# Two q buffers taken in turn, and x0 read back two places later

## The chip, the cores and the metric

One core of a Trainium2 chip runs the whole program. A core has five engines that run their own instruction streams and meet only at semaphores: TensorE (PE in the rows) multiplies matrices, VectorE (DVE), ScalarE (ACT) and GpSimd (POOL) work elementwise, and SyncE (SP) only issues the transfers (DMA) between DRAM and the on-chip memory here. The metric is the device time of one execution in microseconds (us), median of the runs.

## The reference

An attention over pooled keys feeds two feed-forward layers:

```
k_p, v_p = means of k and v over groups of 8 rows       # 8 x 8 heads, 576 rows, 64 wide
attn = softmax(q @ k_p^T / 8);  x = attn @ v_p          # x: 4608 tokens x 512
h = x @ w_in;    g = max(0.01 h, h);         x1  = g @ w_out     # 512 -> 2048 -> 512
h = x1 @ w2_in;  g = h * clip(h+3, 0, 6)/6;  out = g @ w2_out
```

All of it is float32. Each float32 matrix product is made of three products of rounded parts (high by high, high by low, low by high).

## The kernel before, in words

**Tiles, steps and places.** The tokens are cut into 9 tiles of 512 columns for each of the two layers, 18 tiles in all. A tile is worked off in 8 steps, each for two blocks of the hidden layer. The first matrix product of a step (`part`, L1393) is done by seven smaller block products, numbered 0 to 6; the eight matmul groups of the second product (`second`, L1421) that belong to earlier steps lie between them. Each step has 8 places, so a tile has 64. The attention of the next batch runs between these matmuls, at fixed places: tile 0 to tile 6 each carry the four units (pairs of heads) of one batch. A unit's nine stages stand in the table `UNIT_PLACES`: its scores (q times the pooled k) stand second, at the places 3, 15, 27 and 39 for the units 0 to 3; `pv1`, the last, gives the last half of its x0.

**SP's queue.** SP issues all transfers in program order, and waits in order too: a transfer that waits holds all behind it. In an attention tile (`attention_tile`, L509) this order is written out place by place. `stream` (L455) reloads the ring buffer of a weight factor once the product that used it is done, for use two steps later. At LOAD_PLACES `load_unit` (L392) loads k, q and v of the next unit; q's load waits until the scores of the unit before have been multiplied, because all units after the first batch share one q buffer. At STORE_PLACES `store_x0` (L396) stores a unit's x0 to DRAM, and at X_PLACES `load_x0` (L406) reads the columns of the tile to come back into x_stage, after waiting for the store to land. After step 1 `store_y` stores the four banks of the tile before.

**The second layer's weights.** In the tiles 2 to 6 the kernel also prepares the second layer's weight factors, seven in each tile: ScalarE rounds a factor (`factor2_hi`, L873, at places 19 to 25), GpSimd takes the rest (L766), and SP stores it (`store_prep2`, L478, at places 21 to 27). The buffer stage2 has four slots, so that factor 4 uses slot 0 again, once the store of factor 0 has landed:

```
act.wait_ge(prep2_stored[at % SLOTS2], stored2(i, at))
nc.scalar.activation(stage2[:, at % SLOTS2, 0:2], ...)
```

Behind it on ScalarE, in step 3, stands the copy of product 0 out of the accumulator (`p`, L1045), for which product 2 waits on TensorE, since it uses the same bank.

Of the kernel before, what the change touches and what calls it, by code (L numbers as in the profile page):

```python
# [11 lines left out]
P = 128  # L12
# [5 lines left out]
ROWS = 96  # L18
SUB = S // ROWS
HALF_SUB = SUB // 2  # L20
HALF = S // 2
# [28 lines left out]
LOAD_PLACES = (3, 15, 27, 39)  # L50
STORE_PLACES = (16, 28, 40, 51)
X_PLACES = (18, 30, 42, 53)

FIRST_UNIT_PLACES = [(0, 6, 7, 9, 10, 13, 15, 16, 18),
# [3 lines left out]
FIRST_LOAD_PLACES = (6, 19, 30, 41)  # L58
FIRST_STORE_PLACES = (20, 31, 42, 52)
FIRST_X_PLACES = (22, 33, 44, 54)  # L60


SUM_K_PLACES = (52, 10, 22, 34)
# [72 lines left out]
def ffn_attention_kernel(nc, qT, kT, v, w1_in, w1_out, w2_in, w2_out, x0T, x1T, w1_in_split,  # L136
                         w2_in_split, out):
    with ExitStack() as ctx:
        def sb(name, shape, dt=F32):
            return ctx.enter_context(nc.sbuf_tensor(name, shape, dt))  # L140
# [4 lines left out]
        def sem(name):  # L145
            return ctx.enter_context(nc.semaphore(name))
# [7 lines left out]
        def attention_buffers(sb, c, pad=0):  # L154
            def buf(name, shape, dt=F32):
                return sb(name + str(c), shape, dt)
            u = AttentionBuffers()
            if pad:
                buf("pad", [P, pad // 4])
            u.k_raw = buf("k_raw", [P, KEYS, POOL])  # L160
            u.v_raw = buf("v_raw", [KEYS, 2, D, POOL])
            u.q_raw = buf("q_raw", [P, 2, HALF])
            u.k_sum = buf("k_sum", [P, KEYS])
            u.v_sum = buf("v_sum", [KEYS, 2, D])
            u.kT = buf("kT", [P, PAIR_KEYS])
            if c:
                buf("gap", [P, 4 * HALF + PAIR_KEYS])
            u.v_hi = buf("v_hi", [KEYS, 2, P], F32R)
            u.v_lo = buf("v_lo", [KEYS, 2, P], F32R)
            u.prob = buf("prob", [ROWS, 2, HALF_SUB * 2, KEYS])  # L170
            u.row_max = buf("row_max", [ROWS, 2, HALF_SUB * 2])
            u.row_sum = buf("row_sum", [ROWS, 2, HALF_SUB * 2])
            u.row_den = buf("row_den", [ROWS, 2, HALF_SUB * 2])
            u.row_inv = buf("row_inv", [ROWS, 2, HALF_SUB * 2])
            u.pT_hi = buf("pT_hi", [KEYS, 2, HALF], F32R)
            u.pT_lo = buf("pT_lo", [KEYS, 2, HALF], F32R)
            u.x0_stage = buf("x0_stage", [P, 2, HALF])
            return u
# [4 lines left out]
        units = [None] * PAIRS  # L183
# [3 lines left out]
        for c, groups in ((1, (0, 2)), (2, (1, 3))):  # L187
            ring.append(sb(f"ring{c}", [P, PRODUCTS, 4, P], F32R))
            units[c] = overlaid(lambda sb: attention_buffers(sb, c, 4096))
            for group in groups:  # L190
                w_hi = sb(f"wout_hi{group}", [P, ROWS_IN, DM], F32R)
                wout_raw[group] = overlaid(lambda sb: sb(f"wout_raw{group}", [P, ROWS_IN, DM]))
                wout[group] = [w_hi, sb(f"wout_lo{group}", [P, ROWS_IN, DM], F32R)]
        units[3] = overlaid(lambda sb: attention_buffers(sb, 3, 128))
        p1, u2, u3 = (sb(name, [P, HN]) for name in ("p1", "u2", "u3"))
        h = sb("h", [P, 2, N])
# [9 lines left out]
        raw = overlaid(lambda sb: sb("raw", [P, 2, 4, 2, P]))  # L206
        y_stage = sb("y_stage", [P, DC, N])
        units[0] = attention_buffers(sb, 0, 32)
        xp_hi = overlaid(lambda sb: (sb("pad_hi", [P, 3, 2, HN]),
                                     sb("xp_hi", [P, DC, N], F32R)))[1]  # L210
# [15 lines left out]
        def first(b):  # L226
            return isinstance(b, int) and b == 0

        def buffers(b, c):
            return units[c] if first(b) else units[0]  # L230

        def freed(b, c):

            return 0 if first(b) else PAIRS * b + c

        def per_pair(name):
            return [sem(name + str(c)) for c in range(PAIRS)]
# [9 lines left out]
        q_loaded = per_pair("q_loaded")  # L247
# [7 lines left out]
        scores_done = sem("scores_done")  # L255
# [106 lines left out]
        def above_zero(eng, semaphore, value):  # L362

            if not isinstance(value, int) or value > 0:
                eng.wait_ge(semaphore, value)
# [7 lines left out]
        def is_first(T):  # L373
            return isinstance(T, int) and T == 0
# [4 lines left out]
        def _(sp):  # L379
            def load_k_q(b, c):  # L380

                u = buffers(b, c)
                above_zero(sp, k_summed, freed(b, c))
                sp.dma_start(u.k_raw[:], kT[b, c]).then_inc(k_loaded[c], 16)
                above_zero(sp, scores_done, 2 * freed(b, c))
                sp.dma_start(u.q_raw[:], qT[b, c]).then_inc(q_loaded[c], 16)

            def load_v(b, c):
                above_zero(sp, v_summed, freed(b, c))
                sp.dma_start(buffers(b, c).v_raw[:], v[b, c]).then_inc(v_loaded[c], 16)  # L390

            def load_unit(b, c):  # L392
                load_k_q(b, c)
                load_v(b, c)

            def store_x0(b, c):  # L396
                sp.wait_ge(x0_copied, 2 * (PAIRS * b + c) + 2)
                sp.dma_start(x0T[c * P:(c + 1) * P, bass.ds(b * S, S)],
                             buffers(b, c).x0_stage[:].rearrange("p a n -> p (a n)")
                             ).then_inc(x0_stored[c], 16)  # L400
# [87 lines left out]
            def attention_at(T, place, next_unit=True):  # L488
                loads, stores, x_loads = (
                    (FIRST_LOAD_PLACES, FIRST_STORE_PLACES, FIRST_X_PLACES) if is_first(T)  # L490
                    else (LOAD_PLACES, STORE_PLACES, X_PLACES))
                for c in range(PAIRS):
# [41 lines left out]
            sp.wait_ge(first_k_summed, 1)  # L534
            sp.dma_start(units[0].k_raw[:], kT[1, 0]).then_inc(k_loaded[0], 16)
            sp.wait_ge(scores_done, 2)
            sp.dma_start(units[0].q_raw[:], qT[1, 0]).then_inc(q_loaded[0], 16)
            store_x0(0, 0)
            store_x0(0, 1)
            load_piece(0)  # L540
# [306 lines left out]
        def _(act):  # L847
# [39 lines left out]
            def piece_hi(piece):  # L887
                _, raw_w, hi, _ = piece_views(piece)
                act.wait_ge(w_loaded[piece % PIECES], 16 * (piece // PIECES + 1))
                nc.scalar.activation(hi, raw_w, ACT.Copy).then_inc(w_hi_ready, 1)  # L890
# [475 lines left out]
        def _(pe):  # L1366
            def product(acc, left, right, first=True, last=True):

                pe.matmul(acc, left[0], right[0], start=first, stop=False)  # L1369
                pe.matmul(acc, left[0], right[1], start=False, stop=False)  # L1370
                return pe.matmul(acc, left[1], right[0], start=False, stop=last)  # L1371
# [73 lines left out]
            def stage(name, b, c):  # L1445
                u, n = buffers(b, c), 4 * b + c
                if name == "scores":
                    pe.wait_ge(q_loaded[c], 16 * (b + 1))
                    pe.wait_ge(kT_ready, 2 * n + 2)
                    above_zero(pe, x0_copied, 2 * freed(b, c))  # L1450
                    for half in range(2):
                        for at in range(HALF_SUB):
                            mm = pe.matmul(
                                u.ps[0:ROWS, half, at * PAIR_KEYS:(at + 1) * PAIR_KEYS],
                                u.q_raw[:, half, at * ROWS:(at + 1) * ROWS], u.kT[:],
                                start=True, stop=True)
                        mm.then_inc(scores_done, 1)
                if name in ("turn_p0", "turn_p1"):
                    half = int(name[-1])
                    pe.wait_ge(prob_ready, 2 * n + half + 1)  # L1460
                    for hd in ((0, 1), (1, 0))[half]:
                        if half == 1 and hd == 0:
                            pe.wait_ge(x0_copied, 2 * n + 1)
                        for j in range(HALF_SUB):
                            mm = pe.transpose(u.ps[0:KEYS, hd, j * ROWS:(j + 1) * ROWS],
                                              u.prob[:, half, 2 * j + hd, :],
                                              ident[0:ROWS, 0:ROWS])
                    mm.then_inc(p_turned, 1)
                if name in ("pv0", "pv1"):
                    half = int(name[-1])  # L1470
                    pe.wait_ge(pT_ready, 2 * n + half + 1)
                    if half == 0:
                        pe.wait_ge(v_ready, 2 * n + 2)
                    for hd in range(2):
                        mm = product(u.ps[:, half, 0:HALF], (u.v_hi[:, hd, :], u.v_lo[:, hd, :]),
                                     (u.pT_hi[:, hd, :], u.pT_lo[:, hd, :]), hd == 0, hd == 1)
                    mm.then_inc(pv_done, 1)
# [134 lines left out]
```

## Time and profile before

| what | value |
|---|---|
| time, median of 3 runs | 1733.42 us (1729.87 to 1739.12) |
| the profiled execution: time, span | 1732.34 us, 1730.6 us |
| mean granted clock of TensorE | 0.992 |
| TensorE busy | 1691.3 us (98% of the span) |
| VectorE, ScalarE, GpSimd busy | 1024.0, 632.5, 394.1 us |
| DMA | 366.04 MB on SP's queue, 67.3% of 16 engines |

The span runs from the first to the last instruction of the profiled execution. Busy TensorE is not TensorE at its peak, as its matmuls overlap. Attention fills roughly the first 790 us, then tiles run without it.

### The profile page before, as it was taken

To read this page: it belongs to the slowest core of one execution; us is meant where nothing else is said; L and a number is where in the kernel's file an instruction comes from. 1 tells how busy PE (TensorE), PEld (TensorE's weight loads), DVE (VectorE), ACT (ScalarE), POOL (GpSimd) and SP (SyncE) were. 2 spreads that over 40 slices of the span, in tenths; PEclk is the share of its full clock that TensorE was granted. 3 is DMA by queue.
4 is the path that set the end of the run, shared out by engine and by line. 5 is a ranking of instruction groups with operands and counts; after the bars stand their busy time and mean duration, and the time that the engine had idled before them with its cause. 6 is when DMAs were issued, how large, how long until landed. Compare 5 with 4: busy or idle time off the path is not lost. (4 is left out here: it accounts for less than half of the span.)

```text
span 1730.6 us, 33189 instructions
## 1 busy us (share of the span) xinstructions
PE 1691.3 (98%) x10588; PEld 1506.7 (87%) x10588; DVE 1024.0 (59%) x1807; ACT 632.5 (37%) x1329; POOL 394.1 (23%) x427
## 2 busy tenths in 40 slices
PE   7999999999999999999999999999999999999999
PEld 6788888988888888899999888989898888989898
DVE  7767776686766867666454655454544444444444
ACT  4554443333333433333222333333333333333332
POOL 6226542021120212103332202121211112121200
PEclk8999999999999999999999999999999999999999
DMA  7756877667676676767777757575757675757562
GB/s 199 228 159 201 271 249 247 214 201 259 204 243 220 208 247 215 242 196 268 239 258 245 257 172 224 176 220 175 218 170 220 178 219 171 223 173 223 173 197 77
DMA packets 215810, 366.83 MB, mean 212 GB/s; under 512 B 22464, under 2 KB 47040, under 8 KB 215744
## 3 DMA queue, kind: packets, MB, share of 16 engines
q1 hardware_dynamic: 215744, 366.04, 67.3%
q8 instruction: 30, 0.49, 0.1%
q14 instruction: 36, 0.29, 0.0%
HBM read 308.28 MB, written 57.67 MB: 211 GB/s over the span
## 5 line engine op out<-in xcount | busy, mean ns | idle before, releaser
L1416 PE MATMUL ps_h<-xs_hi,ring 128*128 128x256 f32 x3808 | 823.8, 285 | 20.5 <-ACT p L1045 15.9
L1416 PEld LDWEIGHTS ps_h<-xs_hi,ring 128*128 128x128 f32 x3808 | 645.5, 190 | 69.5 <-ACT p L1045 19.8
L1416 PE MATMUL ps_h<-xs_lo,ring 128*128 128x256 f32 x1904 | 537.4, 282 | 0.0
L1416 PEld LDWEIGHTS ps_h<-xs_lo,ring 128*128 128x128 f32 x1904 | 361.2, 190 | 27.0
L931 ACT ACTIVATE g_hi<-gate 128x512 fp32r<-128x512 f32 x288 | 181.9, 632 | 404.6 <-DVE gate L1126 221.8
L1185 DVE TENSOR_TENSOR u<-ps_h,p 128x256 f32<-128x256 f32 x272 | 114.2, 420 | 205.9 <-PE ps_h L1416 155.0
L1369 PE MATMUL ps_y<-g_hi,wout_hi 128*128 128x512 f32 x576 | 229.2, 398 | 0.5 <-DVE y_stage L1181 0.3
L1370 PE MATMUL ps_y<-g_lo,wout_hi 128*128 128x512 f32 x576 | 228.7, 397 | 0.0
L1370 PE MATMUL ps_y<-wout_lo,g_hi 128*128 128x512 f32 x576 | 227.8, 395 | 0.0
L1369 PE MATMUL ps_y<-wout_hi,g_hi 128*128 128x512 f32 x576 | 227.5, 395 | 0.1
L1371 PE MATMUL ps_y<-g_hi,wout_lo 128*128 128x512 f32 x576 | 226.1, 393 | 0.0
L1371 PE MATMUL ps_y<-wout_hi,g_lo 128*128 128x512 f32 x576 | 224.3, 389 | 0.0
L923 ACT ACTIVATE pre<-h,three 128x512 f32<-128x512 f32 x144 | 103.2, 717 | 265.1 <-DVE h L1185 206.6
L1185 DVE TENSOR_TENSOR h<-ps_h,u 128x256 f32<-128x256 f32 x272 | 113.8, 418 | 101.3 <-PE ps_h L1416 100.8
L747 POOL TENSOR_TENSOR xs_lo<-x_stage,xs_hi 128x512 fp32r<-128x512 f32 x30 | 43.9, 1464 | 492.6 <-ACT xs_hi L903 492.6
L1145 DVE SCALAR_TENSOR_TENSOR g_lo<-gate,g_hi 128x512 fp32r<-128x512 f32 x144 | 103.9, 722 | 85.4 <-ACT g_hi L931 85.4
L1132 DVE SCALAR_TENSOR_TENSOR gate<-pre,h 128x512 f32<-128x512 f32 x144 | 109.5, 760 | 66.1 <-ACT pre L923 66.0
L1141 DVE TENSOR_TENSOR g_lo<-gate,g_hi 128x512 fp32r<-128x512 f32 x144 | 106.8, 742 | 62.3 <-ACT g_hi L931 60.7
L1371 PEld LDWEIGHTS ps_y<-g_hi,wout_lo 128*128 128x128 f32 x576 | 108.9, 189 | 24.3
L1371 PEld LDWEIGHTS ps_y<-wout_hi,g_lo 128*128 128x128 f32 x576 | 108.3, 188 | 23.9
L1369 PEld LDWEIGHTS ps_y<-g_hi,wout_hi 128*128 128x128 f32 x576 | 109.4, 190 | 8.8 <-DVE y_stage L1181 0.8
L1126 DVE SCALAR_TENSOR_TENSOR gate<-h 128x512 f32<-128x512 f32 x144 | 108.5, 754 | 13.0 <-ACT h L1007 4.2
(115 smaller groups left out, 2021.4 us busy)
## 6 DMA issues: line engine op xcount, KB each, us to landing
ring<-w_in_split SPq DMA_DIRECT2D x920, 256.0 KB, 2.8
w_in_split<-ring SPq DMA_DIRECT2D x56, 256.0 KB, 3.6
w_in_split<-stage SPq DMA_DIRECT2D x56, 256.0 KB, 4.3
k_raw<-in_kT SPq DMA_DIRECT2D x32, 288.0 KB, 3.4
q_raw<-in_qT SPq DMA_DIRECT2D x32, 288.0 KB, 3.1
v_raw<-in_v SPq DMA_DIRECT2D x32, 288.0 KB
x0T<-x_stage SPq DMA_DIRECT2D x32, 288.0 KB, 4.4
x1T<-y_stage SPq DMA_DIRECT2D x36, 256.0 KB, 3.8
```

The source lines that it names most:

```text
L747: nc.gpsimd.tensor_tensor(xs_lo[:, r], x_block(r), xs_hi[:, r].bitcast(F32), ALU.subtract).then_inc(x_ready, 1)
L923: nc.scalar.activation(pre[:, upper], h[:, upper], ACT.Relu, bias=three[:]).then_inc(pre_ready, 1)
L931: nc.scalar.activation(g_hi[:, g_slot(i, upper)], gate[:, upper], ACT.Copy, scale=1.0 / 6.0 if layer == 2 else 1.0).then_inc(g_hi_ready, 1)
L1126: nc.vector.scalar_tensor_tensor(gate[:, upper], h[:, upper], SLOPE, h[:, upper], ALU.mult, ALU.max).then_inc(gate_ready, 1)
L1132: nc.vector.scalar_tensor_tensor(gate[:, upper], pre[:, upper], 6.0, h[:, upper], ALU.min, ALU.mult).then_inc(gate_ready, 1)
L1141: nc.vector.tensor_tensor(g_lo[:, slot], gate[:, upper], g_hi[:, slot].bitcast(F32), ALU.subtract).then_inc(g_ready, 1)
L1145: nc.vector.scalar_tensor_tensor(g_lo[:, slot], gate[:, upper], 1.0 / 6.0, g_hi[:, slot].bitcast(F32), ALU.mult, ALU.subtract).then_inc(g_ ...
L1185: return nc.vector.tensor_tensor(to, banks[bank], other, ALU.add)
L1369: pe.matmul(acc, left[0], right[0], start=first, stop=False)
L1370: pe.matmul(acc, left[0], right[1], start=False, stop=False)
L1371: return pe.matmul(acc, left[1], right[0], start=False, stop=last)
L1416: mm = pe.matmul(banks[BANK_OF[r]], a, b[:, r, c, :], start=r in OPENS and c == 0 and n == 0, stop=c == 1 and n == 2, skip_group_check=True)
```

## The change

The batch-by-batch units get two q buffers, taken in turn by unit number; with them the load of q waits for the scores of the unit two before instead of those of the unit before. The reload of x0 is placed two places later for the units 0 to 2 of a tile (the last stays at 53). In tile 0 the loads of units move one or two places up, and the reloads of x0 two places down.

```diff
-X_PLACES = (18, 30, 42, 53)
+X_PLACES = (20, 32, 44, 53)
...
-FIRST_LOAD_PLACES = (6, 19, 30, 41)
+FIRST_LOAD_PLACES = (4, 18, 29, 40)
...
-FIRST_X_PLACES = (22, 33, 44, 54)
+FIRST_X_PLACES = (24, 35, 46, 54)
...
-            u.q_raw = buf("q_raw", [P, 2, HALF])
+            u.q_raw = [buf(f"q_raw{i}_", [P, 2, HALF]) for i in range(1 if c else 2)]
...
+        def q_of(b, c):
+            return buffers(b, c).q_raw[0 if first(b) else c % 2]
...
-                above_zero(sp, scores_done, 2 * freed(b, c))
-                sp.dma_start(u.q_raw[:], qT[b, c]).then_inc(q_loaded[c], 16)
+                if not first(b):
+                    sp.wait_ge(scores_done, 2 * (freed(b, c) - 1))
+                sp.dma_start(q_of(b, c)[:], qT[b, c]).then_inc(q_loaded[c], 16)
...
-                                u.q_raw[:, half, at * ROWS:(at + 1) * ROWS], u.kT[:],
+                                q_of(b, c)[:, half, at * ROWS:(at + 1) * ROWS], u.kT[:],
```

SP's queue in tile 6 before, from the q load at place 15 to the first three factor stores (places 21 to 23). x1T is where y is stored, x0T where x0 goes and comes from, w2_in_split takes the factors of the second layer:

```order
L386 DMA q_raw0<-in_qT 128x576 [waits scores_done]
L390 DMA v_raw0<-in_v 72x1024 [waits v_summed]
L470 DMA x1T<-y_stage 128x512 [waits y_copied_act]
L470 DMA x1T<-y_stage 128x512 [waits y_copied_dve]
L470 DMA x1T<-y_stage 128x512 [waits y_copied_act]
L470 DMA x1T<-y_stage 128x512 [waits y_copied_dve]
L452 DMA ring1<-w1_in_split 128x512 [waits product_done] x2
L398 DMA x0T<-x0_stage0 128x576 [waits x0_copied]
L452 DMA ring1<-w1_in_split 128x512 [waits product_done] x2
L403 DMA x_stage<-x0T 128x512 [waits x0_stored0,x_ready]
L452 DMA ring1<-w1_in_split 128x512 [waits product_done] x3
L480 DMA w2_in_split<-stage2 128x512 [waits prep2_ready] x3
```

The same piece of the queue in the changed kernel:

```order
L392 DMA q_raw0_0<-in_qT 128x576 [waits scores_done]
L396 DMA v_raw0<-in_v 72x1024 [waits v_summed]
L476 DMA x1T<-y_stage 128x512 [waits y_copied_act]
L476 DMA x1T<-y_stage 128x512 [waits y_copied_dve]
L476 DMA x1T<-y_stage 128x512 [waits y_copied_act]
L476 DMA x1T<-y_stage 128x512 [waits y_copied_dve]
L458 DMA ring1<-w1_in_split 128x512 [waits product_done] x2
L404 DMA x0T<-x0_stage0 128x576 [waits x0_copied]
L458 DMA ring1<-w1_in_split 128x512 [waits product_done] x4
L409 DMA x_stage<-x0T 128x512 [waits x0_stored0,x_ready]
L458 DMA ring1<-w1_in_split 128x512 [waits product_done]
L486 DMA w2_in_split<-stage2 128x512 [waits prep2_ready] x3
```

Four ring loads instead of two now stand between the store of x0 and its reload, and one instead of three between the reload and the factor stores. The q load has the same place and another value to wait for.

SP's queue at the start of tile 0 before:

```order
L431 DMA w1_in_split<-ring2 128x512 [waits block_ready] x3
L384 DMA k_raw0<-in_kT 128x576 [waits k_summed]
L386 DMA q_raw0<-in_qT 128x576 [waits scores_done]
L390 DMA v_raw0<-in_v 72x1024 [waits v_summed]
L420 DMA raw<-in_moe_w_in 128x2x128 [waits block_ready]
```

And in the changed kernel:

```order
L388 DMA k_raw0<-in_kT 128x576 [waits k_summed]
L392 DMA q_raw1_0<-in_qT 128x576 [waits scores_done]
L396 DMA v_raw0<-in_v 72x1024 [waits v_summed]
L437 DMA w1_in_split<-ring2 128x512 [waits block_ready] x3
L426 DMA raw<-in_moe_w_in 128x2x128 [waits block_ready]
```

The three stores of weight blocks now stand behind the loads of k, q and v.

## Rows read from the trace of the kernel before

**Rows 1.** Busy time by stretch (PE, PEld, DVE, ACT, POOL), granted clock, DMA share, GB/s.

```profile
180.00:283.00 103.00, 101.50 (x664) 89.96 (x663) 79.10 (x137) 41.07 (x100) 47.63 (x56) 1.00 0.77 251
...
283.00:800.00 517.00, 503.26 (x3266) 450.16 (x3265) 361.18 (x660) 181.21 (x426) 84.30 (x109) 0.99 0.71 225
800.00:1731.00 931.00, 922.46 (x5740) 826.70 (x5738) 452.46 (x812) 323.60 (x611) 177.74 (x143) 1.00 0.65 203
```

**Rows 2.** Timeline of PE, the five waits: start, us, instruction, [idle before <-releaser].

```profile
298.94 0.39 PE L1416 MATMUL ps_h<-xs_hi,ring 128*128 128x256 f32 x1 [3.10 <-ACT p L1045]
...
405.15 0.40 PE L1416 MATMUL ps_h<-xs_hi,ring 128*128 128x256 f32 x1 [2.44 <-ACT p L1045]
...
511.54 0.58 PE L1416 MATMUL ps_h<-xs_hi,ring 128*128 128x256 f32 x1 [2.38 <-ACT p L1045]
...
618.36 0.38 PE L1416 MATMUL ps_h<-xs_hi,ring 128*128 128x256 f32 x1 [3.07 <-ACT p L1045]
...
722.78 0.56 PE L1416 MATMUL ps_h<-xs_hi,ring 128*128 128x256 f32 x1 [2.14 <-ACT p L1045]
```

**Rows 3.** Stretches behind the first, fourth and fifth wait: PE busy, clock, DMA.

```profile
299.00:303.00 4.00, 4.00 (x17) 0.57 0.79 284
...
618.00:622.00 4.00, 3.49 (x21) 1.00 0.78 245
722.00:727.00 5.00, 4.21 (x17) 0.66 0.74 239
```

**Rows 4.** Timeline of ACT: the rounding of factors 4 and 5.

```profile
298.20 0.42 ACT L883 ACTIVATE stage<-s_sum 128x256 fp32r<-128x256 f32 x1 [4.03 <-DMA w_in_split<-stage]
...
301.18 0.40 ACT L883 ACTIVATE stage<-s_sum 128x256 fp32r<-128x256 f32 x1
```

**Rows 5.** Timeline of SP's transfers from place 15 to place 23 of tile 2.

```profile
277.20 1.28 SPq L384 DMA_DIRECT2D k_raw<-in_kT  x1
281.11 0.34 SPq L386 DMA_DIRECT2D q_raw<-in_qT  x1
...
282.18 2.27 SPq L470 DMA_DIRECT2D x1T<-y_stage  x4
...
286.53 0.34 SPq L398 DMA_DIRECT2D x0T<-x_stage  x1
287.01 1.11 SPq L452 DMA_DIRECT2D ring<-w_in_split  x2
291.39 0.35 SPq L403 DMA_DIRECT2D x_stage<-x0T  x1
291.86 1.31 SPq L452 DMA_DIRECT2D ring<-w_in_split  x3
293.42 1.54 SPq L480 DMA_DIRECT2D w_in_split<-stage  x3
```

**Rows 6.** Timeline of PE: last matmul of products 5 and 6, transposes before the wait.

```profile
288.10 0.28 PE L1416 MATMUL ps_h<-xs_hi,ring 128*128 128x256 f32 x1
...
290.04 0.28 PE L1416 MATMUL ps_h<-xs_hi,ring 128*128 128x256 f32 x1
...
295.18 0.66 PE L1465 MATMUL ps_att<-ident,prob 96*72 96x96 f32 x6
```

**Rows 7.** Timeline of POOL: the low parts of factor 0, and of factors 1 and 2.

```profile
286.27 0.74 POOL L766 TENSOR_TENSOR stage<-raw_s,stage 128x256 fp32r<-128x256 f32 x1
290.65 1.93 POOL L766 TENSOR_TENSOR stage<-raw_s,stage 128x256 fp32r<-128x256 f32 x2 [3.64 <-ACT stage L883]
```

**Rows 8.** Timeline of DVE: the sum of v at place 13.

```profile
277.59 1.21 DVE L1248 TENSOR_REDUCE v_sum<-v_raw 72x128 f32<-72x1024 f32 x1
```

**Rows 9.** Busy time by stretch, as rows 1.

```profile
280.00:282.00 2.00, 2.00 (x19) 2.00 (x18) 1.49 (x3) 0.18 (x1) 0.00 (x0) 1.00 0.12 44
```

**Rows 10.** Line L480, the factor stores issued at 293.42 and at 300.69: landing times.

```profile
DMA to landing us min/median/max: 4.8/4.8/4.8
...
DMA to landing us min/median/max: 2.9/2.9/2.9
```

More of the change, by code:

```diff
@@ L536, in _ @@
             sp.wait_ge(scores_done, 2)
-            sp.dma_start(units[0].q_raw[:], qT[1, 0]).then_inc(q_loaded[0], 16)
+            sp.dma_start(q_of(1, 0)[:], qT[1, 0]).then_inc(q_loaded[0], 16)
             store_x0(0, 0)
```

## The prediction, made before the changed kernel ran

> **What bounds the kernel now.** I read the stages first, by busy time in stretches [rows 1]. After the attention part (800 to 1731 us) TensorE is busy for 922.5 of 931 us at full clock. The change touches no instruction there, so I take that stretch as fixed. In the attention part TensorE is again what counts: in 180 to 283, one tile's length, it is idle for 1.5 us of 103; in 283 to 800, five tiles' length, for 13.7 us of 517, at a mean clock of 0.99. ScalarE and VectorE are far from full there. So only a wait that TensorE itself feels, or a lowered clock, is worth time.
>
> Then I read what TensorE waits for between 283 and 800 us. There is one long wait in each of the five tiles 2 to 6, always at the same point: the first matmul of product 2 in step 3 of the tile waits for ScalarE's copy p (L1045): 3.10, 2.44, 2.38, 3.07 and 2.14 us [rows 2]. These are 13.1 of the 13.7 us. Behind the first wait, the clock is granted at 0.57 for 4 us, that is three of four microseconds near the lower level (1.2 instead of 2.4 GHz), a loss of 4 x 0.43 = 1.7 us. Behind the second and third the rows read the same (three such in all); behind the fifth 5 us show 0.66 (5 x 0.34 = 1.7 us); behind the fourth, though it was one of the longest, the clock stayed at 1.00 [rows 3]. Four losses of 1.7 are 6.8 us. The place is worth 13.1 + 6.8 = 19.9 us.
>
> Why is p late? ScalarE runs in order, and ahead of p it rounds factor 4 of the second layer's weights into a slot of stage2 (L883). Four slots serve seven factors, so factor 4 needs slot 0, whose old content must have been stored to DRAM. ScalarE is idle for 4.03 us until that store has landed, at 298.20; then it rounds, copies p, then TensorE at 298.94 [rows 4]. Had the store landed 3.10 us earlier, at 295.10, TensorE would not have waited: its transposes before it end at 295.84 [rows 6].
>
> Why does the store land late? Its data were ready at 287.01 (GpSimd, 286.27 + 0.74) [rows 7], but SP issued it only at 293.42 [rows 5], over six microseconds later. SP's queue says why. At place 15 it issues k at 277.20, and the next instruction, q, only at 281.11: it waits for the scores of the unit before, at the same place in TensorE's order. It then pushes v and four y stores, so ring loads and the store of x0 follow late and bunched: x0's store goes out at 286.53. Two ring loads later, SP meets the reload of x0, which waits for that store; it stands until 291.39. Only then come three ring loads in a row, whose products had all ended by 290.32 (290.04 + 0.28) [rows 6], and then the store that ScalarE needs.
>
> **The change part by part.**
> *Two q buffers.* The load of q now waits for the scores of the unit two before, which lie twelve places back, some 19 us at 103 us for 64 places. At place 15 SP gets q out right behind k, near 278.6 instead of 281.11. The v load needs the sum of the v before it, which is placed at 13; that sum ends at 278.80 (277.59 + 1.21) [rows 8], so v goes near 279. Then y (2.27 us; its last bank is copied in step 1 as well, at place 10) to about 281.7, the first two ring loads of step 2, and the x0 store near 283.5 instead of 286.5, its data being copied behind place 14. The transfers don't crowd: in 280 to 282 the DMA engines are busy only 0.12 of the time now [rows 9]. No instruction is added on any engine; SP has the same count of transfers. In the Fori loop two register operations move, and none of TensorE's do.
> *The x0 reload two places later* (18 to 20). SP issues the ring loads of products 3, 4 and 5 as they end, and meets the reload after product 5, whose matmuls end at 288.38 [rows 6]. The x0 store, out at 283.5, has then had 4.9 us; in before it took no more than 4.9 us (286.53 to 291.39 [rows 5]). So the wait is about nothing. The reload goes at 288.8; its data aren't needed before all four pieces are there, and the fourth stays at place 53, so this costs nothing. The ring load of product 6 then waits for its product, 290.32, takes 0.1 + 0.36 us, and the factor store follows 0.25 us behind (as from 291.86 + 1.31 to 293.42 in [rows 5]): 291.0 instead of 293.42, that is 2.4 us earlier. It can't be earlier, since product 6 stands ahead of it.
> *When it lands.* In before the landing took 4.8 us, behind one x0 load and three ring loads issued in 2 us; a later store of the same size with little ahead of it took 2.9 us [rows 10]. The two ends are landings at 293.9 and at 295.8. By the first nothing is left of the wait. By the second 295.8 - 295.1 = 0.7 us is left in each of the two tiles with a 3.1 us wait and none in the other three: 1.4 us. I take a point between, 0.5 us in all, since two instead of four transfers stand just ahead.
> The Trainium skill (DMA: Bandwidth & Descriptors, section Queues, rings and completion order) speaks against this part: the increment of a semaphore is a strongly ordered write, which lands only after every earlier write of the same DMA engine. The trace agrees in kind: 4.8 us with a queue ahead and 2.9 us with little. By this rule the reload, now right ahead of the factor store, is itself part of its landing, which pulls toward the longer of my two ends.
> *The same move in units 2 and 3 (30 to 32, 42 to 44) and the earlier q* free SP of waits too, but ring loads are issued two steps (over 20 us) before their use and TensorE waits for none of them, so I count 0. If that cover were gone, every microsecond of a late ring load would show on TensorE.
> *Tile 0.* Loads of k, q, v come one or two places earlier, one set now ahead of three weight stores instead of behind; the x0 reloads go two places later. TensorE has no SP-fed wait there. 0, bounded by +-2 us, the size of the idle time before 283.
> *Behind the wait.* With the pause gone, factors 5 and 6 need slots 1 and 2. Factor 1 is ready in GpSimd before 292.6 [rows 7], its store goes out near 292, and even at 4.8 us it lands before 297; ScalarE reaches factor 5 at 301.18 now [rows 4], less 3.1 us that is 298.1. So no stall follows there.
>
> **Sum.** The waits 13.1 - 0.5 = 12.6, the clock 6.8: 19.4 us. The profiled execution took 1732.34 us (span 1730.6), 1 us under the median of the runs, 1733.42; I predict 1732.3 - 19.4, rounded to 1713 us. By the bounds: 18.5 us to 19.9 us, and +-2 us for tile 0 and the luck of the clock.
>
> **The rivals.**
> *Half of it.* The store lands 5 to 6 us after its issue because reload, ring load and the traffic moved forward are still under way. With 0.8 us more than the 4.8, the waits left are 1.5, 0.8, 0.8, 1.5 and 0.5 us, 5.1 us in all, and if the clock still falls behind them as before, only 8.0 us are won: 1724 us. For it: DMA share near full in this stretch now. Against it: that share is high because SP pushes a backlog, which the change spreads.
> *Nothing.* SP is held by something else behind q (the v sum, the y copies, or ring products), or the store is not what p waits for: 1732 us. Against it: SP's queue runs nearly without pause from 281.11 to 288.1, so it was working off a backlog.
> *Slower.* The pause is where ScalarE and VectorE catch up. Without it, the softmax chain of the following units (probabilities, turned and split) comes late for TensorE at the places 25 to 60. Each such wait would cost what one of today costs, about 2.6 + 1.4 = 4 us. One new wait per tile gives the gain back (5 x 4 = 20 us, no change); from two per tile on it is slower, by 20 us: 1753 us. For it: VectorE is busy 361 of 517 us, in bursts. Against it: the stretch 180 to 283 has the same softmax work and no such pause, VectorE is busy for 79.1 of its 103 us, and TensorE is idle for 1.5 us [rows 1].
>
> **How the numbers follow.** Forecast (1713, own range 1709 to 1719): 0.76. Half: 0.11, split between faster and same. Nothing, or gain given back: 0.08. Slower: 0.05. Within 0.5% (8.7 us) a measurement of this kernel can't tell a change. Faster 0.76 + 0.08 = 0.84, same 0.11, slower 0.05. The range reaches from 1708 (all of the 19.9 us, 2 us of tile 0, and a better draw of the clock) to 1727.
>
> **What would show it.** On SP: q right behind k at places 3, 15, 27, 39; no wait over 1 us at the x0 reload of unit 0; the first factor store 2 to 2.5 us after where TensorE's product 5 ends, not 5. On ScalarE: the wait of factor 4 for the store under 1 us. On TensorE: no wait for p over 1 us in tiles 2 to 6, and their mean clock 1.00. Tiles 2 to 6 should take about 4 us less each, all else the same. I am wrong if the factor store is issued early and ScalarE still waits for its landing, or if TensorE's waits come back on the turned probabilities.

## The result, and the profile after

The changed kernel takes 1713.67 us, median of 4 runs (1712.43 to 1718.73), against 1734.09 us for the kernel before: a ratio of 0.9887, 95% interval 0.9853 to 0.992. The forecast was 1713. Timed again later beside other kernels it took 1714.41 us, ratio 0.9878 (0.9858 to 0.9899).

The stretches of the changed kernel (columns as in [rows 1]):

```profile
250.00:800.00 550.00, 548.54 (x3601) 490.58 (x3600) 401.56 (x726) 199.40 (x466) 103.10 (x128) 1.00 0.74 234
800.00:1717.00 917.00, 908.68 (x5655) 814.28 (x5653) 443.70 (x800) 320.08 (x602) 169.90 (x135) 1.00 0.65 202
```

The same first stretch of the kernel before:

```profile
250.00:800.00 550.00, 535.87 (x3478) 479.08 (x3477) 388.52 (x708) 193.36 (x452) 89.89 (x115) 0.99 0.70 224
```

TensorE's idle time there fell from 14.1 to 1.5 us and the clock is full. The five waits of [rows 2] are gone. All that the list of waits gives for TensorE between 250 and 800 us, in the kernel after:

```profile
PE ps_h L1422 <- DVE h L1191: 0.9, 3, 0.3
```

(0.9 us in three waits, the longest 0.3.) SP's queue at place 15 to 21 of tile 2, as in [rows 5]:

```profile
282.99 0.75 SPq L388 DMA_DIRECT2D k_raw<-in_kT  x1
283.93 0.34 SPq L392 DMA_DIRECT2D q_raw<-in_qT  x1
284.62 0.33 SPq L396 DMA_DIRECT2D v_raw<-in_v  x1
285.23 2.52 SPq L476 DMA_DIRECT2D x1T<-y_stage  x4
287.91 1.24 SPq L458 DMA_DIRECT2D ring<-w_in_split  x2
289.41 0.34 SPq L404 DMA_DIRECT2D x0T<-x_stage  x1
289.90 4.63 SPq L458 DMA_DIRECT2D ring<-w_in_split  x4
294.87 0.35 SPq L409 DMA_DIRECT2D x_stage<-x0T  x1
296.15 0.32 SPq L458 DMA_DIRECT2D ring<-w_in_split  x1
296.73 0.34 SPq L486 DMA_DIRECT2D w_in_split<-stage  x1
```

And ScalarE at the same place, as in [rows 4]:

```profile
299.43 0.54 ACT L959 ACTIVATE kT<-k_sum 64x72 f32<-64x72 f32 x2
300.23 0.42 ACT L889 ACTIVATE stage<-s_sum 128x256 fp32r<-128x256 f32 x1 [0.26 <-DMA w_in_split<-stage]
300.55 0.36 ACT L1051 ACTIVATE p<-ps_h 128x256 f32<-128x256 f32 x1
```

In this execution the tile lies 5.79 us later than in the profile before (k at 282.99 instead of 277.20). With that taken off, q goes out at 278.1, the x0 store at 283.6, the reload at 289.1 without a wait of note, and the factor store at 290.9 instead of 293.42. It lands 3.5 us later (300.23 - 296.73), and ScalarE waits for it 0.26 us instead of 4.03.

The 5.79 us come from the prologue, and they hide a part of the gain in the profiled pair (1718.73 against 1732.34 us, 13.6 us apart). Counted from the load of k at place 15 of tile 2 to the end of the span, the pair is 1730.6 - 277.20 = 1453.4 and 1716.9 - 282.99 = 1433.9 us: 19.5 us apart. The first 75 us, before, then after, then in the run with the late reload alone (further down), whose program is that of before up to tile 1:

```profile
0.00:75.00 75.00, 61.64 (x360) 53.24 (x361) 53.27 (x86) 36.50 (x81) 36.68 (x68) 0.91 0.72 214
```

```profile
0.00:75.00 75.00, 62.18 (x334) 54.48 (x335) 52.36 (x84) 34.71 (x75) 31.87 (x64) 0.82 0.68 218
```

```profile
0.00:75.00 75.00, 62.24 (x334) 54.58 (x335) 52.52 (x84) 34.72 (x75) 31.94 (x64) 0.82 0.70 214
```

TensorE is busy about as long, at a lower clock: 75 x 0.09 = 6.8 us less of full-speed time. SP's order in the changed kernel differs from about 48 us on (tile 0), but the third line shows the same low clock with the order of before, and tile 2 lies 4.99 us late there too. So it is in the main a matter of the single execution; the section on surprises has more of them.

### The profile page after: what moved, and what is told of

The parts are those of the page before. It is cut to its first block and busy times, and to the rows that moved or that the text cites. A ratio compares the mean times of both kernels' runs of the same rounds, so it can differ in the third digit from the quotient of the medians.

```text
span 1716.9 us, 33189 instructions
## 1 busy us (share of the span) xinstructions
PE 1690.1 (98%) x10588; PEld 1505.8 (88%) x10588; DVE 1026.2 (60%) x1807; ACT 632.3 (37%) x1329; POOL 395.4 (23%) x427
## 5 line engine op out<-in xcount | busy, mean ns | idle before, releaser
L1132 DVE SCALAR_TENSOR_TENSOR gate<-h 128x512 f32<-128x512 f32 x144 | 108.7, 755 | 13.7 <-ACT h L1013 4.9
```

The costliest lines, as they stand in the source:

```text
L1132: nc.vector.scalar_tensor_tensor(gate[:, upper], h[:, upper], SLOPE, h[:, upper], ALU.mult, ALU.max).then_inc(gate_ready, 1)
```

## The experiments

My theory: product 6 and SP's position in its queue decide when the store of factor 0 goes out; that store decides when ScalarE rounds factor 4; and the copy p behind it decides whether TensorE waits. Rivals: the reload alone counts; the traffic, not the issue, makes the landing late; the gain comes from elsewhere. The executions of a kernel spread over 2 to 13 us, so medians are compared by their ratios to the runs of before that they share.

**The two q buffers alone.** The edit is against the changed kernel; it sets all three tables of places back to those of before.

```diff
-X_PLACES = (20, 32, 44, 53)
+X_PLACES = (18, 30, 42, 53)
...
-FIRST_LOAD_PLACES = (4, 18, 29, 40)
+FIRST_LOAD_PLACES = (6, 19, 30, 41)
...
-FIRST_X_PLACES = (24, 35, 46, 54)
+FIRST_X_PLACES = (22, 33, 44, 54)
```

> The two q buffers alone, every place as in the kernel before. Queue theory: SP gets q, v and y out 2.5 us earlier at place 15, the store of x0 goes out near 3 us earlier and has landed some 3 us earlier, so the reload at place 18 frees SP by about 288.4 (before: 291.39), the ring loads of products 4 and 5 go at once, product 6 sets the factor store, which is issued about 2.4 us earlier: all of the gain of the full change, about 19 us (1714). Rival, that moving the reload is what counts: less than 6 us (over 1727), with TensorE's five waits for p still over 1.5 us each.

Measured 1716.36 us, ratio 0.988 (0.9863 to 0.9898): the gain of the full change within what can be told. SP:

```profile
288.24 0.34 SPq L404 DMA_DIRECT2D x0T<-x_stage  x1
288.72 1.10 SPq L458 DMA_DIRECT2D ring<-w_in_split  x2
292.55 0.35 SPq L409 DMA_DIRECT2D x_stage<-x0T  x1
293.01 1.78 SPq L458 DMA_DIRECT2D ring<-w_in_split  x3
295.05 2.18 SPq L486 DMA_DIRECT2D w_in_split<-stage  x3
```

SP still stands at the reload, from 289.8 to 292.55, but that ends early enough: product 6 is what it waits for last, and the store goes out 2.5 us earlier than before, by the tile's own time (this tile lies 4.12 us later). It lands 4.4 us behind its issue, ScalarE waits 1.19 us for it, and TensorE's waits for p are 0.5 us in all the tiles together.

**The late reload alone.** The edit is against the kernel before.

```diff
-X_PLACES = (18, 30, 42, 53)
+X_PLACES = (20, 32, 44, 53)
```

> One q buffer; the reloads of x0 two places later in the tiles 1 to 6 (20, 32, 44), tile 0 as before. Queue theory: SP is still behind until 288.1, sends two more ring loads, then stands at the reload until the x0 store lands at 291.4, and issues the first factor store near 292.3, 1.1 us earlier. The five waits shrink by 1.1 us each, 5.5 us in all, to 2.0, 1.3, 1.3, 2.0, 1.0; if the clock still falls behind them about 1727, if it no longer does, 1721. Rival, that moving the reload carries the gain: 1714.

Measured 1727.93 us, ratio 0.9945 (0.9927 to 0.9963). The five waits for p are smaller, not gone:

```profile
302.38 0.39 PE L1416 MATMUL ps_h<-xs_hi,ring 128*128 128x256 f32 x1 [1.55 <-ACT p L1045]
...
407.11 0.39 PE L1416 MATMUL ps_h<-xs_hi,ring 128*128 128x256 f32 x1 [2.01 <-ACT p L1045]
...
512.37 0.39 PE L1416 MATMUL ps_h<-xs_hi,ring 128*128 128x256 f32 x1 [1.69 <-ACT p L1045]
...
617.55 0.39 PE L1416 MATMUL ps_h<-xs_hi,ring 128*128 128x256 f32 x1 [1.53 <-ACT p L1045]
...
721.04 0.38 PE L1416 MATMUL ps_h<-xs_hi,ring 128*128 128x256 f32 x1 [1.09 <-ACT p L1045]
```

They are 7.9 us in all where 7.6 were expected. The store goes out at 296.76, which is 291.8 by the times of before (this tile lies 4.99 us later): 1.6 us earlier where 1.1 was expected, and it lands 4.9 us behind its issue. The clock fell behind the second and the third wait only (stretches behind the second, the third and the fifth; PE busy, clock, DMA):

```profile
408.00:412.00 4.00, 4.00 (x18) 0.61 0.49 160
513.00:517.00 4.00, 4.00 (x17) 0.57 0.75 214
...
723.00:727.00 4.00, 3.91 (x26) 1.00 0.84 248
```

Two losses near 1.7 us remain of four. They stand behind the two longest waits of this run (2.01 and 1.69 us), but both waits are shorter than the one of 3.07 us in the kernel before behind which the clock stayed full [rows 3]. Each part of the change works on the same wait, so their gains, by the ratios 0.0120 x 1735 = 20.8 us and 0.0055 x 1735 = 9.5 us, don't add up: both together give 20 us.

**The reload behind the factor stores, one q buffer.** The edit is against the kernel before.

```diff
-X_PLACES = (18, 30, 42, 53)
+X_PLACES = (24, 30, 42, 53)
```

> One q buffer; only the first reload of x0 of a tile is moved, from place 18 to 24, behind the first four factor stores; q still waits for the scores of the unit before. Queue theory: nothing stands between SP and the factor store but the products, so it goes out near 291.0 although q, v and y leave as late as before: 1714, waits for p under 0.7 us. Rival, that the burst of q, v, y and ring transfers (DMA share near 1.0 from 284 to 290) makes the store land late whenever it is issued: the landing takes over 6 us and less than half of the gain is seen (over 1724).

Measured 1715.04 us, ratio 0.9877 (0.986 to 0.9894). One number of one table does what the whole change does. q still waits for its scores and y leaves late, and yet:

```profile
283.96 0.34 SPq L386 DMA_DIRECT2D q_raw<-in_qT  x1
...
289.95 3.58 SPq L452 DMA_DIRECT2D ring<-w_in_split  x5
293.79 2.18 SPq L480 DMA_DIRECT2D w_in_split<-stage  x3
```

The store goes out 2.5 us earlier than before (this tile lies 2.86 us later). It lands 4.7 us behind its issue (ScalarE rounds factor 4 at 298.52), so the traffic does lengthen the landing, as it did before (4.8 us, [rows 10]); it doesn't cost the gain. The rival needed over 6 us. TensorE's waits for p are 0.7 us in all. Medians can't tell this kernel or the one with q alone from the changed one. The single profiles hint at a rest: from the load of k at place 15 of tile 2 to the end of the span they take 1435.7 and 1436.5 us, the changed kernel 1433.9 and, timed again, 1432.9.

**The stores taken off SP's queue.** ScalarE issues all seven of a tile at the same places; q and x0 are untouched. The edit is against the kernel before.

```diff
-                if 0 <= place - STORE2_PLACE < PRODUCTS:
-                    store_prep2(i, place - STORE2_PLACE)
...
+                        if attention and 0 <= at < PRODUCTS:
+                            act.wait_ge(prep2_ready, PRODUCTS * eighth + at + 2)
+                            act.dma_start(factor_rows(w2_in_split, eighth, PREP_ORDER[at]),
+                                          flat(stage2[:, at % SLOTS2])
+                                          ).then_inc(prep2_stored[at % SLOTS2], 16)
```

> The kernel before with q and x0 untouched; the seven factor stores of an attention tile are issued by ScalarE instead of SP, at the same places 21 to 27, so that SP's queue no longer holds them. Queue theory: the first goes out near 291.7 instead of 293.42 and overtakes what SP holds; waits for p shrink by at least 1.7 us each, 1718 to 1724 with ScalarE's added issue time of seven stores a tile. Rival, that SP's queue is not what makes the store late: 1733.

Measured 1712.47 us, ratio 0.9861 (0.9841 to 0.9881), better than the 1718 to 1724 that I expected. ScalarE has the store out at 292.12, which is 290.1 by the times of before (its tile lies 2.00 us later), while SP still stands:

```profile
292.12 0.40 ACTq L1041 DMA_DIRECT2D w_in_split<-stage  x1
```

```profile
288.90 1.10 SPq L452 DMA_DIRECT2D ring<-w_in_split  x2
293.32 0.35 SPq L403 DMA_DIRECT2D x_stage<-x0T  x1
```

I had put the issue at 291.7. SP's long waits at q and at the reload are all still there in this kernel (67.0 and 74.3 us in all) and cost nothing: they mattered through the stores queued behind them.

**The stall put back.** The changed kernel, with the store of factor 0 alone held back behind two ring loads.

```diff
-                if 0 <= place - STORE2_PLACE < PRODUCTS:
+                if place == STORE2_PLACE + 3:
+                    store_prep2(i, 0)
+                if 0 < place - STORE2_PLACE < PRODUCTS:
```

> The changed kernel, with only the store of factor 0 moved behind the first two ring loads of step 3 (place 24), so that SP must first see product 1 of that step. Queue theory: it goes out at about 295.3 in the times of before, lands 3.5 to 4.8 us later, and ScalarE's wait and TensorE's wait for p come back at 3.7 to 5.0 us in each of five tiles, 18 to 25 us, with 1.7 us of lowered clock behind four or five of them: 1739 to 1747, although both q buffers and the late reload are in place. Rival, that the change won its time elsewhere (earlier loads, fewer stalls of SP in general): it stays under 1725.

Measured 1741.93 us, ratio 1.0037 (1.0023 to 1.0052): slower than the kernel before. ScalarE, and SP's load of k and its store behind the ring loads:

```profile
301.75 0.42 ACT L891 ACTIVATE stage<-s_sum 128x256 fp32r<-128x256 f32 x1 [4.86 <-DMA w_in_split<-stage]
```

```profile
279.93 1.33 SPq L388 DMA_DIRECT2D k_raw<-in_kT  x1
...
296.67 1.05 SPq L458 DMA_DIRECT2D ring<-w_in_split  x2
297.92 1.86 SPq L486 DMA_DIRECT2D w_in_split<-stage  x2
```

TensorE waits 17.6 us for p in five waits (3.94, 3.11, 3.72, 3.67, 3.16), a little under the 18 to 25 expected, and all five have a lowered clock behind them; behind the first, third and fourth it stays low longer (the first three stretches: PE busy, clock, DMA):

```profile
302.00:309.00 7.00, 6.51 (x26) 0.55 0.44 113
410.00:417.00 7.00, 6.33 (x32) 0.76 0.45 132
517.00:525.00 8.00, 6.95 (x31) 0.60 0.38 129
```

That is 7 x 0.45 = 3.2, 7 x 0.24 = 1.7 and 8 x 0.40 = 3.2 us of full-speed time. Read in slices of 1 us, with the edges, the five losses are 3.4, 1.7, 3.4, 3.4 and 1.7, 13.7 us in all.

The store goes out at 295.2 by the times of before (this tile lies 2.73 us later), as expected (295.3). Waits and clock add up to 31.3 us here and to 19.9 before, 11.4 us more; from the load of k to the end of the span it takes 1742.1 - 279.93 = 1462.2 us, 8.8 more than before. So one late store takes back the whole gain, and the rest of the change can be worth no more than some 2 or 3 us in this pair of profiles.

**Tile 0 as before**, the rest changed. The edit is against the changed kernel.

```diff
-FIRST_LOAD_PLACES = (4, 18, 29, 40)
+FIRST_LOAD_PLACES = (6, 19, 30, 41)
...
-FIRST_X_PLACES = (24, 35, 46, 54)
+FIRST_X_PLACES = (22, 33, 44, 54)
```

> The changed kernel with the places of tile 0 as before; this tells whether tile 0's part is worth anything. I costed it at 0 within 2 us: 1714, the same as the changed kernel. Rival: tile 0's loads matter, and it differs by over 2 us.

Measured 1716.39 us, ratio 0.9892 (0.9877 to 0.9908), beside 0.9887 and 0.9878 of the changed kernel: no difference that the intervals show. Whether tile 0's part is worth 1 or 2 us stays open.

**Both q buffers, reload at place 24.** The edit is against the changed kernel.

```diff
-X_PLACES = (20, 32, 44, 53)
+X_PLACES = (24, 32, 44, 53)
```

> The changed kernel with the first reload of a tile at place 24 instead of 20, behind the factor stores. Theory: product 6 sets the store's issue in either case, and only about 0.45 us of SP's time for the reload goes; the changed kernel has no wait of TensorE for p left to win, so 1713 to 1715. Rival, that the reload directly ahead lengthens the landing of the store enough to be felt: 2 us or more faster.

Measured 1715.08 us, ratio 0.9882 (0.9863 to 0.9901): nothing more to win, as expected. The store, issued at the same moment of the tile, lands 3.0 us later instead of 3.5, and ScalarE doesn't wait for it at all.

**All of the change, and ScalarE's stores.** The edit is that of the run with ScalarE's stores, on the changed kernel.

> The changed kernel with the factor stores of the attention tiles issued by ScalarE, at their places, as in the run with one q buffer. TensorE has about 1.5 us idle between 250 and 800 us in either kernel, so nothing is left to win: 1712 to 1714, no more than 1 us from the better of the two. Rival: freeing SP and moving the stores add up, under 1710.

Measured 1711.49 us, ratio 0.9862 (0.9844 to 0.988). By their ratios both kernels with ScalarE's stores (0.9861 and 0.9862) looked some 4 us better than the changed one (0.9887), each beside its own runs of before, so the three were timed side by side.

> The changed kernel itself, unedited, timed again beside the two versions in which ScalarE issues the factor stores, so that the three share one chip and one set of runs of the kernel before. By the theory, with TensorE idle for 1.5 us between 250 and 800 us: 1713 to 1716, a ratio near 0.988.

> The kernel before with its factor stores issued by ScalarE, again. If its first 1712.5 was no chance it stays 2 to 3 us below the changed kernel; by the theory, with the same idle time on TensorE, the two are equal within 1.5 us.

> The changed kernel with its factor stores issued by ScalarE, again. By the theory equal within 1.5 us to the changed kernel; if the two edits add up or ScalarE's issuing helps by itself, 2 us or more below it.

Measured, in this order: 1714.41 us, 0.9878 (0.9858 to 0.9899); 1713.1 us, 0.9872 (0.9849 to 0.9895); 1712.78 us, 0.9867 (0.9845 to 0.9889). The order is the same as the first time and the differences are 1.3 and 1.6 us, within the intervals. From the load of k in tile 2 to the end of the span, the four profiles with ScalarE's stores take 1431.6 to 1432.5 us, the two of the changed kernel 1433.9 and 1432.9, which hints at 1 us. I can't say that a version beats the changed kernel.

## Why the prediction was right

*What bounds.* Right: the part after attention has 8.3 us idle in 917 where it had 8.5 in 931. The five places of [rows 2] with the clock behind them held 19.9 us, and from tile 2 on the profiled pair is 19.5 us apart.

*The q load.* Predicted at 278.6, v at 279, the x0 store at 283.5; they came at 278.1, 278.8 and 283.6. SP's waits moved on as named: in 250 to 800 us it still waits 5.9 us for sums of v, in nine short waits.

*The reload.* Right that no wait of note is left before it in tile 2 and that it costs nothing where it is. What the step didn't say, and the runs showed, is that this half isn't needed once q goes early: alone, q's part gives the full gain, and the reload's part about half of it (7.9 of 13.1 us of waiting stay). In the sum I let both work together, which was right for the forecast but tells nothing of the shares.

*The store's issue.* Predicted 291.0; it came at 290.9, and at 290.9 too in the runs with q alone and in both with the reload at 24. Four ways to free SP end at the same instant, since product 6 stands ahead in the queue in each. That is the strongest sign that the bound was named rightly.

*Its landing.* The ends were 2.9 and 4.8 us; it took 3.5 us in tile 2. With this, TensorE's waits for p fell to nothing where I had left 0.5 us. The Trainium skill (DMA: Bandwidth & Descriptors, section Queues, rings and completion order) has the semaphore wait for earlier writes of the same DMA engine; the trace agrees in kind, with 4.4 and 4.7 us in the runs where ring loads are bunched ahead (three in 1.78 us, five in 3.58 us). The reload right ahead goes with a longer landing, as the prediction had it by this rule, but by little: 3.5, 3.7 and 3.9 us in the three profiles with both q buffers and the reload there, 3.0 us where it stands at place 24. What stands right ahead isn't all: with the late reload alone the same two transfers, the reload and one ring load, are right ahead, and it took 4.9 us. The DMA share was 1.02 between 294 and 296 us of that run, with the issue at 296.76, against 0.80 in the same stretch of the changed kernel, with the issue at 296.73. That this backlog makes the difference is argued from these rows, not shown by a run.

*The clock.* Priced at 6.8 us: between 250 and 800 us no lowered stretch is left. 14.1 - 1.5 = 12.6 us of idle time and 6.8 us of clock are 19.4 us, the forecast sum to the tenth; by the ratio the gain is 1734.09 x 0.0113 = 19.6 us. That agreement is partly luck: the interval of the ratio allows some 14 to 25 us, and the price was read from one profile of before, in which the clock fell in four places of five. The mean clock of that execution was 0.992; in the executions of before beside the experiments it lay between 0.986 and 0.994, and 0.001 of the span is 1.7 us.

*The rivals.* Half of it: no. The landing was shorter, not longer. Nothing: no. Slower: no, VectorE and ScalarE had no chain that came late, 1.5 us of idle time in 550 us, 0.9 us of it in the three waits for VectorE above. Tile 0: not told from 0.

SP's waits for q and for the reload in the kernel before, all places together (us in total, times, longest). The wait for x0T is filed under two lines, that of the wait (L409) and that of the load (L403):

```profile
SPq L386 <- PE ps_att L1453: 67.7, 23, 11.4
SPq L409 <- DMA x0T<-x_stage: 49.7, 20, 4.9
...
SPq L403 <- DMA x0T<-x_stage: 16.4, 8, 2.9
```

And what is left of them in the changed kernel:

```profile
SPq L415 <- DMA x0T<-x_stage: 13.0, 12, 2.6
...
SPq L409 <- DMA x0T<-x_stage: 1.9, 2, 1.8
...
SPq L392 <- PE ps_att L1459: 1.7, 5, 0.4
```

Together they fell from 133.8 us to 16.6 us, and that was worth 20 us only through the store behind. SP now waits elsewhere: its waits for TensorE's products rose from 809.2 to 878.0 us. And with one q buffer and the reload at place 24 it still waited 73.1 us for q and 51.0 us for x0, with the gain all there.

## What to carry to other kernels

Find the wait that the bounding engine feels, then walk back through the in-order queues until an instruction was ready long before it was issued: here a store ready at 287.0 was issued at 293.4, behind two waits of other transfers. Only a wait of SP with something urgent behind it is worth removing; the kernel before has 67.7 us of q waits in all, and of these, by the order of the queue, just the one at place 15 of five tiles took part in costing time. Moving one entry past the urgent transfer can do what another buffer does.

## What the runs showed that I had not expected

A wait costs more than itself, and not in proportion: behind waits of 2.1 to 3.1 us the clock fell in four cases of five, behind 1.1 to 2.0 us in two of five, behind 3.1 to 3.9 us in five of five, where the three longest (3.67 to 3.94 us) lost 3.4 us each and the other two 1.7 us. Behind a wait of 3.07 us it once stayed full [rows 3].

The prologue is a draw. In the kernels with one q buffer, whose programs are the same in this stretch, the mean clock of the first 75 us was 0.91, 0.82, 0.86, 0.91 and 0.91 (before, the late reload alone, the reload at 24, ScalarE's stores twice); in the changed kernel it was 0.82 and, timed again, 0.84. One tenth of it is 7.5 us, near the whole gain that the rival "half of it" would have left (8.0 us), so a pair of profiles compares tiles well and totals badly. Counted from tile 2 on, the two profiles of the changed kernel are 1.0 us apart.
